# Early attention units and the first dense chunk of a fused attention and expert kernel in another order, without dummy products

## The reference, cut to what matters

```
q, k, v: (4 batches, 8 heads, 576, 64)
pooled attention over groups of 4 rows (q_d, k_d, v_d are means over 4):
    out_up    = repeat(softmax(q_d k_d^T / 8) v_d, 4)
local attention, |i - j| < 4:
    out_local = softmax(masked q k^T / 8) v
x = out_up + out_local                          # 2304 tokens x 512
h = x @ w_in                                    # 512 -> 2048
g = h where h >= 1; 0 where h <= -1; else (h + 1)^2 / 4
y = g @ w_out                                   # 2048 -> 512
logits = y @ w_gate                             # 8 experts, 288 tokens each
each token goes to one expert, in order of its logits: relu(y @ w1[e]) @ w2[e]
```

## Time and profile before

| | us |
|---|---|
| median of 3 runs | 869.7 (867.36 to 869.98) |
| profiled execution | 869.2 |
| its span, first to last instruction | 867.4 |
| mean granted TensorE clock | 0.973 |
| TensorE busy | 820.8 (95%) |
| VectorE, ScalarE, GpSimd busy | 509.9, 406.8, 333.2 |

### The profile page before, as it was taken

The page is one execution under the profiler, slowest core; times in us unless marked ns, Lnnn a source line. Parts: engine busy times, 40 slices in busy tenths (PEclk is TensorE's granted clock), DMA queues, the critical chain, the costliest instruction groups (busy, mean ns, idle before and its releaser), DMA issues. The chain is left out here.

```text
span 867.4 us, 21161 instructions
## 1 busy us (share of the span) xinstructions
PE 820.8 (95%) x7658; PEld 748.8 (86%) x7658; DVE 509.9 (59%) x1424; ACT 406.8 (47%) x1006; POOL 333.2 (38%) x391
## 2 busy tenths in 40 slices
PE   6779999999999999999999999939999999999995
PEld 4668889898889898898999999838999999999995
DVE  4667776655665665563544344366766766766620
ACT  4555655445545553553444444303454454455461
POOL 6570233113302321240000000007687787787882
PEclk9898999999999999999999999957999999999998
DMA  9975421320321333201101000006625625616611
GB/s 198 245 195 153 121 88 45 91 79 22 92 80 44 67 90 80 67 2 39 49 2 49 0 24 2 22 4 222 220 68 185 233 61 202 229 49 219 219 40 45
DMA packets 99301, 85.49 MB, mean 99 GB/s; under 512 B 63664, under 2 KB 71856, under 8 KB 99248
## 3 DMA queue, kind: packets, MB, share of 16 engines
q1 hardware_dynamic: 93808, 74.74, 29.6%
q0 software_dynamic: 3072, 9.44, 3.7%
q10 hardware_dynamic: 2368, 0.59, 0.4%
HBM read 70.60 MB, written 14.16 MB: 98 GB/s over the span
## 5 line engine op out<-in xcount | busy, mean ns | idle before, releaser
L528 PE MATMUL PS<-xs,W 128*128 128x256 f32 x1728 | 234.5, 285 | 1.3 <-DVE xT L432 1.3
L528 PEld LDWEIGHTS PS<-xs,W 128*128 128x128 f32 x1728 | 222.9, 189 | 12.5 <-issue 3.1
L528 PE MATMUL PS<-W,g 128*128 128x512 f32 x864 | 221.3, 394 | 1.5 <-DVE g L660 1.5
L528 PEld LDWEIGHTS PS<-W,g 128*128 128x128 f32 x864 | 153.2, 188 | 30.0 <-DVE g L660 3.2
L633 ACT ACTIVATE scratch<-PS,minus 128x256 f32<-128x256 f32 x144 | 68.4, 475 | 215.3 <-DVE scratch L670 215.3
L670 DVE TENSOR_SCALAR scratch<-PS 128x256 f32<-128x256 f32 x144 | 61.0, 424 | 124.5 <-PE PS L528 123.6
L441 POOL TENSOR_TENSOR P<-P,top 128x640 f32<-128x640 f32 x11 | 13.9, 1262 | 220.8 <-DVE top L391 220.8
L1549 POOL TENSOR_TENSOR w1s<-w1r,w1s 128x512 fp32r<-128x512 f32 x64 | 80.8, 1289 | 28.5 <-ACT w1s L1437 28.2
L1344 PE MATMUL PS<-exs,w1s 128*128 128x288 f32 x256 | 81.2, 317 | 0.0
L1344 PE MATMUL PS<-ehs,w2s 128*128 128x288 f32 x256 | 80.9, 316 | 0.0
L1345 PE MATMUL PS<-exs,w1s 128*128 128x288 f32 x256 | 76.3, 298 | 0.0
(11 more groups left out here) (198 smaller groups left out, 1445.8 us busy)
## 6 DMA issues: line engine op xcount, KB each, us to landing
w1r<-in_moe_w SPq DMA_DIRECT2D x16, 1024.0 KB, 5.0
w2r<-in_moe_w SPq DMA_DIRECT2D x16, 1024.0 KB
vd<-in_v SPq DMA_DIRECT2D x16, 288.0 KB
xt<-xT SPq DMA_DIRECT2D x16, 288.0 KB, 2.2
y<-scratch SPq DMA_DIRECT2D x18, 256.0 KB, 2.1
vw<-in_v SPq DMA_DIRECT2D x34, 128.0 KB, 2.8
scratch<-in_moe_w_in SPq DMA_DIRECT2D x8, 512.0 KB, 5.8
scratch<-in_moe_w_out SPq DMA_DIRECT2D x8, 512.0 KB, 5.1
```

The costliest lines, as they stand in the source:

```text
L528: r = pe.matmul(psum, wsel(w[i]), xsel(x[j]), start=first and t == 0, stop=last and t == 2)
```

## The change

The loop over the early units, the whole of chunk 0 and the units 4 to 6 in it are written out call by call, on every engine, in an order that no longer follows units and steps. To that end functions are split: `dve_centre` into `dve_top` and `dve_centre`, `dve_rden` into `dve_den` and `dve_rden`, `pool_probs` into `pool_p` and `pool_pd`, the chunk's step into `pe_layer1`, `pe_layer2`, `act_relu`, `act_square`, `act_g` and `dve_clip`. From chunk 1 on every engine does the same operations in the same order as before. `FIRST_PLAN` goes, and so do the dummy products of the early units. The pieces of W_in and W_out come alternately, and GpSimd splits seven of the 16 instead of four. The core of the diff:

```diff
 INNER = DM * FF // 128 // PIECE
-ORDER = [0, 1, 2, 3, 4, 5, 6, 8, 9, 10, 11, 7, 12, 13, 14, 15]
-POOL_PIECES = [1, 3, 5, 6]
-LATER_PIECES = [2, 4, None, None]
-BY_POOL = sorted(POOL_PIECES)
+ORDER = [0, 1, 8, 2, 9, 3, 10, 4, 11, 5, 12, 6, 13, 7, 14, 15]
+BY_POOL = [2, 5, 8, 9, 11, 12, 14]
 BY_DVE = [i for i in range(ALL) if i not in BY_POOL]
-CHUNK_PIECES = {0: 7, 1: 8, 2: 9, 3: 10, 4: 11, 8: 12, 9: 13, 10: 14, 11: 15}
 SLOT_OF = [i % SLOTS for i in range(ALL)]
...
 
+        def dve_top(dve, n, T):
+            dve.wait_ge(scores, n + 1)
+            dve.tensor_reduce(top[:, :, :], both(T, G * KB).rearrange("p h (g k) -> p g h k", k=KB), AX.X, ALU.max).then_inc(top_ready, 1)
+
         def dve_centre(dve, n, T):
-            dve.wait_ge(scores, n + 1)
+            dve.wait_ge(top_ready, n + 1)
             s = both(T, G * KB)
-            link(dve, dve.tensor_reduce(top[:, :, :], s.rearrange("p h (g k) -> p g h k", k=KB), AX.X, ALU.max), top_ready, n + 1)
             dve.tensor_tensor(P[:, :, :, :].rearrange("p g h k -> p h g k"), s.rearrange("p h (g k) -> p h g k", k=KB),
                               top[:, :, :].rearrange("p g h -> p h g").unsqueeze(3).to_broadcast([128, 2, G, KB]),
...
+        def dve_den(dve, n, T):
+            dve.wait_ge(exp_done, n + 1)
+            dve.tensor_reduce(PS[:, T, 500:500 + 2 * G], P[:, :, :, :].rearrange("p g h k -> p (g h) k"),
+                              AX.X, ALU.add).then_inc(den_done, 1)
+
         def dve_rden(dve, n, T):
-            dve.wait_ge(exp_done, n + 1)
+            dve.wait_ge(den_done, 2 * n + 1)
             den = PS[:, T, 500:500 + 2 * G]
-            link(dve, dve.tensor_reduce(den, P[:, :, :, :].rearrange("p g h k -> p (g h) k"),
...
             each = 1 if small else G
             for a in range(0, G, each):
@@ -458,6 +461,8 @@
                 x = pool.tensor_tensor(p, p, rden[:, a:a + each, :].rearrange("p g h -> p (g h)").unsqueeze(2).to_broadcast([128, 2 * each, KB]),
                                        ALU.mult)
             x.then_inc(probs, 1)
+
+        def pool_pd(pool, n, small=True):
...
+                load_q(sp, 0, (0,))
+                load_k(sp, 0, (0,))
+                load_q(sp, 1, (0,))
+                load_k(sp, 1, (0,))
+                load_vd(sp, 0)
+                load_piece(0)
+                load_piece(1)
+                sp.wait_ge(heads_turned, 2)
+                load_k(sp, 2)
+                load_vw(sp, 0, 0)
+                sp.wait_ge(heads_turned, 1)
+                load_q(sp, 2)
+                load_piece(2)
+                sp.wait_ge(vp_ready, 1)
+                load_vd(sp, 1)
+                load_gate()
+                load_vw(sp, 1, 1)
+                sp.wait_ge(heads_turned, 4)
+                load_k(sp, 3)
+                load_piece(3)
+                store_x(0)
+                sp.wait_ge(heads_turned, 3)
+                load_q(sp, 3)
+                sp.wait_ge(vp_ready, 2)
+                load_vd(sp, 2)
+                sp.wait_ge(att_out, 2)
+                load_vw(sp, 2, 0)
+                load_piece(4)
+                sp.wait_ge(heads_turned, 5)
+                load_q(sp, 4)
+                store_x(1)
+                sp.wait_ge(att_out, 3)
+                load_vw(sp, 3, 1)
+                sp.wait_ge(heads_turned, 6)
+                load_k(sp, 4)
+                sp.wait_ge(vp_ready, 3)
+                load_vd(sp, 3)
+                load_piece(5)
...
-                for n in range(EARLY):
-                    pool_vp(pool, n)
-                    if n:
-                        rest_of_first_x(pool, n - 1)
-                    pool_probs(pool, n, small=False)
-                    pool_piece(pool, POOL_PIECES[n])
-                pool.wait_ge(xs_lo, EARLY)
-                pool_vp(pool, EARLY)
-                pool_probs(pool, EARLY)
-                with pool.Fori(EARLY + 1, UNITS) as n:
+                pool_vp(pool, 0)
+                pool_p(pool, 0, small=False)
+                pool_pd(pool, 0, small=False)
+                pool_p(pool, 1, small=False)
+                pool_pd(pool, 1, small=False)
+                pool_vp(pool, 1)
+                pool_piece(pool, 2)
+                pool_p(pool, 2, small=False)
+                pool_vp(pool, 2)
+                pool_pd(pool, 2, small=False)
+                pool_p(pool, 3, small=False)
+                rest_of_first_x(pool, 1)
+                pool_pd(pool, 3, small=False)
+                pool_vp(pool, 3)
+                pool_piece(pool, 5)
+                pool_p(pool, 4)
+                pool_pd(pool, 4)
+                pool_vp(pool, 4)
+                pool_vp(pool, 5)
+                pool_piece(pool, 8)
+                pool_piece(pool, 9)
+                pool_centre(pool, 5)
+                pool_pd(pool, 5)
+                pool_piece(pool, 11)
+                pool_p(pool, 5)
...
                 act_qT(act, 0, AT[0])
                 act_kT(act, 0, AT[0])
+                act_exp(act, 0)
+                act_qT(act, 1, AT[1])
+                act_kT(act, 1, AT[1])
+                act_expd(act, 0, AT[0])
                 act_piece(act, 0)
-                for n in range(EARLY):
-                    T, other = AT[n % 2], AT[1 - n % 2]
-                    if n:
-                        act_od(act, n - 1, other)
-                    act_exp(act, n)
-                    if n:
-                        act_first_x(act, n - 1)
-                    act_qT(act, n + 1, other)
-                    act_kT(act, n + 1, other)
-                    act_expd(act, n, T)
-                    act_pT(act, n, T)
-                    act_piece(act, POOL_PIECES[n])
-                    act_pdT(act, n, T)
-                    if LATER_PIECES[n] is not None:
-                        act_piece(act, LATER_PIECES[n])
-                act_od(act, EARLY - 1, AT[(EARLY - 1) % 2])
-                act_exp(act, EARLY)
-                act_first_x(act, EARLY - 1)
-                act_expd(act, EARLY, TM)
-                act_chunk(act, 0, FIRST_PLAN, first=True)
+                act_pT(act, 0, AT[0])
+                act_pdT(act, 0, AT[0])
+                act_exp(act, 1)
+                act_od(act, 0, AT[0])
...
+                dve_pool_q(dve, 0)
                 dve_pool_k(dve, 0)
-                dve_pool_q(dve, 0)
+                dve_top(dve, 0, AT[0])
                 dve_centre(dve, 0, AT[0])
+                dve_dtop(dve, 0, AT[0])
+                dve_den(dve, 0, AT[0])
+                dve_rden(dve, 0, AT[0])
+                dve_pool_q(dve, 1)
+                dve_pool_k(dve, 1)
+                dve_rdend(dve, 0)
+                dve_pT(dve, 0, AT[0])
+                dve_top(dve, 1, AT[1])
+                dve_centre(dve, 1, AT[1])
+                dve_dtop(dve, 1, AT[1])
+                dve_den(dve, 1, AT[1])
+                dve_rden(dve, 1, AT[1])
+                dve_xT(dve, 0, AT[0])
                 dve_piece(dve, 0)
-                for n in range(EARLY):
-                    T, other = AT[n % 2], AT[1 - n % 2]
-                    if n > 1:
-                        dve.wait_ge(xs_lo, n - 1)
-                    if n:
-                        dve_xT(dve, n - 1, other)
-                    dve_dtop(dve, n, T)
-                    dve_rden(dve, n, T)
-                    dve_pool_k(dve, n + 1)
-                    dve_pool_q(dve, n + 1)
...
                 pe_scores(pe, 0, AT[0], onto=True)
                 pe_dscores(pe, 0, AT[0])
-                for n in range(EARLY):
-                    T, other = AT[n % 2], AT[1 - n % 2]
-                    if n:
-                        pe_warm(pe, other + 3, WARM_TURN)
-                    pe_turn_qk(pe, n + 1, other, n - 1 if n else None)
-                    if n:
-                        pe_warm(pe, T + 1, WARM_SCORES)
-                    pe_mask(pe, n + 1, other)
-                    pe_scores(pe, n + 1, other, onto=True)
-                    pe_turn_p(pe, n, T)
-                    pe_dscores(pe, n + 1, other)
-                    pe_out_local(pe, n, T, n // 2, n % 2, 0, HALF)
-                    pe_turn_pd(pe, n, T)
-                    pe_out_local(pe, n, T, n // 2, n % 2, HALF, NB)
-                    pe_out_pooled(pe, n, T)
+                pe_turn_qk(pe, 1, AT[1], None)
+                pe_mask(pe, 1, AT[1])
+                pe_scores(pe, 1, AT[1], onto=True)
+                pe_dscores(pe, 1, AT[1])
+                pe_turn_p(pe, 0, AT[0])
+                pe_turn_pd(pe, 0, AT[0])
+                pe_out_local(pe, 0, AT[0], 0, 0, 0, HALF)
+                pe_out_local(pe, 0, AT[0], 0, 0, HALF, NB)
+                pe_out_pooled(pe, 0, AT[0])
+                pe_turn_qk(pe, 2, AT[0], 0)
+                pe_turn_p(pe, 1, AT[1])
+                pe_mask(pe, 2, AT[0])
+                pe_scores(pe, 2, AT[0], onto=True)
+                pe_turn_pd(pe, 1, AT[1])
+                pe_out_local(pe, 1, AT[1], 0, 1, 0, HALF)
```

(30 more changed lines are left out.)

526 lines of the change are left out of this document (399 added, 127 removed).

## The result

The changed kernel took 871.8 us (median of 17 runs, 869.4 to 875.0), the kernel before 868.7 in the same comparison (17 runs, 866.4 to 871.3): a ratio of 1.0041, 95% interval 1.0031 to 1.0052. The forecast was 855.5. The profiled execution took 871.8 us, with a span of 870.1 (867.4 before).

What follows compares the result with a forecast made beforehand. TensorE's dense work was taken to bound the kernel from chunk 1 on. Savings of 6.6 (early part), 5.6 (start of chunk 0) and 1.8 (its rest), 14.0 us, took 869.2 or 869.7 to about 855.5 us; range 850.5 to 865.

Steps and rivals of the forecast that it cites:

- What bounds the kernel: From chunk 1 on (125.69 us) only TensorE binds; any shift of chunk 1's start reaches the end one for one.
- Unit 0: First early unit: its sum on VectorE comes 3.1 us earlier, at 20.3 us; bounds 2.0 and 3.6.
- I keep 9.14 for a unit: Early units: 9.14 us from sum to sum, since the chain through P gets no shorter.
- The dummy products and the clock: Early units: removing the dummies costs 0.9 us through half clock; bounds nothing and 8 us.
- The second rival: Clock lost without dummies: early part ends at 56.5 to 57, only chunk 0 gains; 862 us, chance 0.15.
- Start of chunk 0: Up to the first layer-2 step: 9.7 us against 15.31, P ready as the second step ends; 5.6 us saved.
- I find no step whose wait would be late by over 0.2 us: Rest of chunk 0: the new order adds no late wait; half the loss comes back, 1.8 us saved.
- 3.3 lost: Rest of chunk 0 in the kernel before: 3.3 us of its 53.25 counted as lost.
- The bound of 5 us lost: Rest of chunk 0: the worst case allowed, 5 us lost, against 3.3 saved at best.
- the fifth, no change: Whole kernel: the gains are real but equal to the added waits; 867 to 872 us, chance 0.05.
- the third, a late item in a written-out queue: Chunk 0: a late piece or load stops TensorE and eats chunk 0's gain; 862 to 864 us, chance 0.13.
- My rival for slower: Half clock reaches into chunk 0, 1.3 us more per step; eight steps make it 0.3% slower; chance 0.05.

Runs made afterwards that it cites:

- again: The changed kernel run once more, unaltered: 872.6 us, ratio 1.0073 to the kernel before.
- a_turn: The changed kernel with TensorE's turns of P(5) and P(6) one dense step later, their copies moved along: 874.3 us, ratio 1.0071 to the kernel before.
- a_early: The changed kernel with four early steps moved (q(3)'s load, two x subtractions, VectorE's pieces 3 and 4): 871.9 us, ratio 1.0051 to the kernel before.
- a_dve_pieces: The changed kernel with GpSimd's five pieces of chunk 0 split by VectorE instead: 868.6 us, ratio 1.0003 to the kernel before.
- c2: The changed kernel with all late pieces on VectorE, the four moved steps of a_early and dummy products: 868.1 us, ratio 1.0008 to the kernel before.
- h_new_old: The changed kernel's early part, then chunk 0 in the old order, all nine late pieces on VectorE: 866.9 us, ratio 1.0005 to the kernel before.
- b_lock: The kernel before, order kept, with five of its nine late pieces subtracted on GpSimd instead of VectorE: 867.9 us, ratio 1.0006.
- a_vp: The changed kernel with GpSimd's v sums for unit 5 moved behind pieces 8 and 9: 873.1 us, ratio 1.0049 to the kernel before.

## Why the prediction was wrong, step by step

**What bounds the kernel** was right: the time at which chunk 1 begins goes through to the end, within the scatter of the tail (740.8 us behind it in the changed kernel, 741.7 before).

**Unit 0** was right, 20.84 for 20.3. Its store went out at 24.07 us for 22.5 to 23, and the sum of unit 1 came at 31.18 for 30 to 31; but that number was luck, for the sum did not wait for the store. VectorE was behind, with a subtraction held for 1.66 us by GpSimd.

**"I keep 9.14 for a unit"** was near only as a sum, and only at full clock. I had 18.3 us for units 2 and 3 together; they took 23.3 in the changed kernel's profile and 20.4 in again, but 18.2 in a_turn (32.38 to 50.59), the one execution whose clock was full from 30 us on. That 18.2 meets 18.3 is luck too: unit 2 took 12.1 us there and unit 3 took 6.1. Neither is 9.14.

**The dummy products and the clock** I put at 0.9 us, with 8 as a bound. That is the mis-sized term of the early part: 5.1 us for units 2 and 3 (23.3 against 18.2), and the first dense product at 55.37 where I had 50.5. The second rival, 56.5 to 57 with all units at half clock, was nearer. But the dummies are not the reason: taken out of the kernel before, they cost 0.5 us, inside the interval; put into the changed one they gained about 1, also inside, and the granted clock from 40 to 50 us was 0.52 all the same. I had argued against that rival that TensorE would hardly be idle at half clock, and that the clock would so come back. The first half came true and the second didn't: from 48 to 53 us TensorE was busy for 5.00 of 5.00 us, at a clock of 0.50. a_early's moves cut unit 2 to 12.7 us at partly half clock, so some of it was also what they moved, the pieces on VectorE ahead of the sum among them.

**Start of chunk 0**: 11.51 us for 9.7. The product P is not ready as the second step ends; TensorE waits for it 2.02 us, with no wait for Pd behind it. The kernel before has 2.16 and 0.97. Since the early part ended 4.9 us later than forecast as well, chunk 0's first stretch began and ended late.

**"I find no step whose wait would be late by over 0.2 us"** is the step that failed, and it made the sign: 9.2 us lost in the rest of chunk 0 where I had 1.8 saved. It failed in three ways.

First, GpSimd's pieces. I had laid out the durations of the earlier trace rows, 2.36 and 1.23 us, as if each engine kept its own wherever it was put. With its own numbers: seven pieces on GpSimd instead of four, at 2.36 each, were booked as GpSimd's time alone. They took VectorE's too, and TensorE waited for what VectorE had behind them. Each of the five pieces relieves VectorE of 1.2 us and holds it for (15.1 - 5.1) / 5 = 2.0, going by a_dve_pieces; in the kernel before, (9.7 - 4.4) / 5 = 1.06, which is about even. That is 4.5 us of the 9.2 (62.4 against 57.9 us with the five on VectorE), and more than the 3.1 us by which the changed kernel is slower.

Second, the new order itself has late steps. Without those pieces on GpSimd TensorE still waits 1.94 and 1.33 us ahead of P(5) and P(6), and the rest takes 57.9 us for the 53.4 of the old order behind the same early part. GpSimd's product P(5) alone lasts 3.44 us beside VectorE's pieces there, 2.20 in the kernel before. What the order saves in its first stretch it gives back here: 69.5 and 68.6 us for all of chunk 0 in a_dve_pieces and c2, 68.1 in h_new_old. Which place in the order sets these 4.5 us is open; moving the turns later brought nothing.

Third, there was less to take back than I booked. The earlier trace rows has TensorE busy for 52.03 of the 53.25 us, so that at most 1.2 us of waits could go; the other 2 of my "3.3 lost" were products that took longer than in my sum. The bound of 5 us lost was passed as well.

**The rivals.** By the number the fifth, no change, was nearest: 867 to 872, for gains that the added waits eat up, here 5.6 us against 9.2. By the mechanism it was the third, a late item in a written-out queue: TensorE does stop for what GpSimd's pieces hold up, though by way of VectorE. But I had priced it at a gain of chunk 0 forgone, since I saw one such item and not a mechanism that recurs with each piece. My rival for slower had the half clock reaching into chunk 0 for eight steps; it did so for about three microseconds, as a consequence.

## What to carry to other kernels

Before work is moved between VectorE and GpSimd, look in the trace for the same instruction with and without the other engine beside it: where a mean of several durations hides a 0.4 and a 2.6, treat the two engines as one resource for such instructions, and book the work against the one that the products wait for. Here a wait removed by moving one instruction came back at the next one while that engine's sum stayed the same, so compare the sum over the stretch first and single waits after. Cut the stretch where the clock changes, too: a loss of 2 us in b_lock was hidden by 2 us of clock ahead of it. And where the granted clock differs between executions of the same kernel, read a short stretch from several executions before an order is credited or blamed for it.

## What the runs showed of the hardware that I had not expected

One VectorE instruction can be held for several of GpSimd's in a row: 4.95, 5.39 and 4.01 us in three executions of this order, with the two pieces queued back to back, while in a_vp VectorE got in between the same two and was held 2.38 and 2.27 us. Which of the two it is, I can't say. GpSimd's instruction is stretched likewise when VectorE is there first, P from 1.26 to 2.12 us. And the granted clock of an identical early part was full in two executions from 40 to 50 us, half in three (0.50), and between them in the others.
